# Experts chosen digit by digit beside their matmuls: two matmul pieces per digit step, one-hots shared with GpSimd, owners as one number

## What is computed

```python
logits = x @ w_gate                      # x: [3072, 512], 8 experts
order = np.argsort(-logits.flatten())    # all (token, expert) pairs, best first
for idx in order:
    tok, e = (int(idx) // E, int(idx) % E)
    if assigned[tok] >= 0 or counts[e] >= cap:      # cap = 384
        continue
    assigned[tok] = e
    counts[e] += 1
for e in range(E):
    mask = assigned == e
    h = np.maximum(x[mask] @ w1[e], 0.0)            # w1: [8, 512, 1024]
    out[mask] = h @ w2[e]                           # w2: [8, 1024, 512]
```

## Time and profile before

| | |
|---|---|
| median of 3 runs | 1100.49 us (1099.84 to 1103.88) |
| the profiled execution, its own time | 1108.83 us |
| its span | 1106.7 us |
| busy: TensorE, VectorE, ScalarE, GpSimd | 939.8, 584.7, 320.9, 217.8 us |
| chain that ended last: TensorE, VectorE, issue | 65%, 20%, 7% |

### The profile page before, as it was taken

How to read it: one execution, slowest core, us unless ns; L and a number is a source line. 1 busy time by engine, 2 the same in 40 slices (tenths; PEclk the granted TensorE clock), 3 DMA queues, 4 the chain that set the end, 5 groups by cost and what they waited for, 6 DMA issues and landing times.

```text
span 1106.7 us, 22036 instructions
## 1 busy us (share of the span) xinstructions
PE 939.8 (85%) x7642; PEld 772.7 (70%) x7643; DVE 584.7 (53%) x1683; ACT 320.9 (29%) x651; POOL 217.8 (20%) x294
## 2 busy tenths in 40 slices
PE   5899999816999999999998433989898989898995
PEld 4787878704788888888887322868676767676984
DVE  5756666577222222222221377777777777776650
ACT  3454444406122222222222003132222222224330
POOL 5633433001111111111111001020202020202011
PEclk9999999857999999999999655899899989999998
DMA  9667583704011111111110113141405050507210
GB/s 192 134 133 147 132 166 76 205 24 171 30 38 38 38 38 38 38 38 38 38 38 29 24 52 130 48 154 46 166 23 189 16 195 11 200 12 283 89 48 29
DMA packets 46014, 97.85 MB, mean 88 GB/s; under 512 B 7248, under 2 KB 19584, under 8 KB 45952
## 3 DMA queue, kind: packets, MB, share of 16 engines
q1 hardware_dynamic: 27200, 59.55, 18.5%
q0 software_dynamic: 8064, 26.46, 7.5%
q10 hardware_dynamic: 10688, 11.01, 4.7%
HBM read 77.49 MB, written 19.51 MB: 88 GB/s over the span
## 4 chain that ended last, share of the span: by engine, by line
PE 65%; DVE 20%; issue 7%; ACT 2%; DMA 2%; POOL 2%; DVEq 0%; ACTq 0%; SPq 0%; POOLq 0%
PE bank L766 25%; PE bank L905 9%; PE bank L920 8%; PE bank L678 4%; PE bank L659 3%; DVE w_low L1635 3%; PE bank L719 2%; PE bank L696 2%; PE bank L790 2%; PE bank L668 2%; DVE slot_hot L1614 2%; PE bank L813 2%; PE bank L928 1%; DVE ge L1511 1%; PE bank L856 1%
## 5 line engine op out<-in xcount | busy, mean ns | idle before, releaser
L905 PE MATMUL bank<-xh,w_high 128*128 128x384 f32 x256 | 96.7, 378 | 7.2 <-DVE xl L1639 7.2
L626 POOL DMA_INDIRECT out<-y_second,idx x24 | 35.4, 1475 | 316.2 <-ACT y_second L1049 313.3
L766 PE MATMUL bank<-w_high,xh 128*128 x200 | 82.8, 414 | 10.5 <-DVE gates L1398 10.5
L766 PE MATMUL bank<-w_high,hh 128*128 x200 | 83.1, 416 | 8.7 <-DVE hl L1405 8.7
L905 PE MATMUL bank<-xh,w_low 128*128 128x384 f32 x256 | 87.6, 342 | 0.0
L905 PE MATMUL bank<-xl,w_high 128*128 128x384 f32 x256 | 87.4, 342 | 0.0
L1049 ACT ACTIVATE w_high<-w_landed 128x1024 fp32r<-128x1024 f32 x64 | 63.9, 1049 | 72.1 <-DMA w_landed<-in_moe_w 72.1
L920 PE MATMUL bank<-w_high,hh 128*128 128x512 f32 x192 | 83.7, 436 | 0.0
L766 PE MATMUL bank<-w_low,hh 128*128 x200 | 80.7, 404 | 0.0
L766 PE MATMUL bank<-w_high,hl 128*128 x200 | 80.5, 402 | 0.0
L766 PE MATMUL bank<-w_low,xh 128*128 x200 | 80.2, 401 | 0.0
(11 more groups left out here) (288 smaller groups left out, 1962.3 us busy)
## 6 DMA issues: line engine op xcount, KB each, us to landing
w_landed<-in_moe_w SPq DMA_DIRECT2D x16, 2048.0 KB, 11.3
va<-in_v_win SPq DMA_DIRECT2D x16, 585.0 KB, 6.0
raw_w<-in_moe_w SPq DMA_DIRECT2D x4, 2048.0 KB, 11.9
k_raw<-in_k SPq DMA_DIRECT2D x16, 384.0 KB, 8.8
q_eye<-in_q ACTq DMA_DIRECT2D x16, 384.0 KB, 7.1
x_rows<-x ACTq DMA_DIRECT2D x12, 384.0 KB, 9.8
x_rows<-x SPq DMA_DIRECT2D x4, 387.0 KB, 7.5
xg<-x_rows,gidx POOLq DMA_INDIRECT x26, 3.4
```

The costliest lines, as they stand in the source:

```text
L626: pool.indirect_dma_start(out=out[:, :], out_offset=bass.IndirectOffsetOnAxis(ap=idx2[:, col:col + 1], axis=0), in_=y2[t][:, :], in_offset ...
L766: last = mm(ps, lhs[a][:, c, :], rhs[b](c), start=c == 0 and t == 0, stop=c == n - 1 and t == 2)
L905: last = mm(bank[fc % 2][:, 0:CAP], w[:, q % 2, c, f], a[:, c, :], start=c == 0 and t == 0, stop=c == KC - 1 and t == 2)
```

## The change

- Every search step and every piece of the tail gets two matmul pieces (SEGS = [2] * 12). The last two up chunks of an expert (HEAD = 4 pieces) run at the head of the next phase, ahead of its down pieces. A down part waits only for the weight unit it reads. List and turns move to steps 3 and 4/5; the weights' low units are spread anew, three of them into the tail.
- `slot_hot` is made half by VectorE (`pick_early`, in step 1) and half by GpSimd (`pick_late`, twelve operations of 128x128); the list waits for both.
- `oh`, `free` and the 192-wide products on them go. `owner` holds the number of a token's expert (-1 for none), `gone` is 0 for a free token and 16 for one that is not, and is added to `ix`, so that `cb` comes out zero.
- From step 3 on `known` is no longer updated: the thresholds' digits hold the difference to the digit before, and `nxt` is made from `thr`.

```diff
-DOWNS = 12
-LIST_AT, TURN_AT = 1, 2
-LOWS_AT = [[], [0, 1], [2, 3], [4], [5], [6], [7], []]
-PRE = 3
-SEGS = [3, 3, 3, 2, 2, 2, 2, 2, 1, 2, 2, 1]
+HEAD = 4
+DOWNS = HEAD + 12
+LIST_AT, TURN_AT = 3, 5
+LOWS_AT = [[], [], [0], [1], [2], [3], [], [4]]
+SEGS = [2] * 12
...
+            def pick_late(r):
+                pool.wait_ge(places_ready, r + 1)
+                if r:
+                    pool.wait_ge(listed, r)
+                for j in range(TC // 2, TC):
+                    last = g.tensor_scalar(slot_hot[:, j, :], iota_l[:, :], mlo[:, j:j + 1], None, ALU.is_equal)
+                last.then_inc(late_picks, 1)
+
             for ph in range(1, E + 2):
                 q, r = ph - 2, ph - 1
+                if r < E:
+                    pick_late(r)
...
             def list_mine(r):
                 pe.wait_ge(picks_ready, r + 1)
+                pe.wait_ge(late_picks, r + 1)
...
-                    if t == 0:
-                        pe.wait_ge(low_done, (W1U + W2U) * (q + 1))
...
                 if t == 0:
+                    pe.wait_ge(low_done, (W1U + W2U) * q + W1U + part + 1)
...
+                    elif q >= 0 and k >= HEAD:
+                        outward(q, (k - HEAD) // 4, k % 4)
                     elif q >= 0:
-                        outward(q, k // 4, k % 4)
+                        hidden(q, FC - HEAD // 2 + k // 2, k % 2)
...
+            def prepare_rest(ph):
+                chain(stt(eq3[:, :, :], eq3[:, :, :], -8.0, iota_e8[:, :, :], ALU.mult, ALU.add))
+                chain(red(ix[:, :], eq3[:, :, :], AXX, ALU.min))
+                chain(tt(ix[:, :], ix[:, :], gone[:, :], ALU.add))
+                chain(tt(cb[:, :, :], iota_e[:, :, :], ix[:, :].unsqueeze(2).to_broadcast([P, TC, E]), ALU.is_equal))
...
-                if t >= 2:
+                if t == 2:
                     chain(stt(known[:, :], digit[:, :], 4 * (t - 1) - 3, known[:, :], ALU.logical_shift_right, ALU.bitwise_xor))
...
+                stt(tied[:, :], ix[:, :], m1[:, 0:1], eqt[:, :], ALU.is_equal, ALU.mult).then_inc(tied_ready, 1)
...
-                chain(tt(oh[:, :, :], oh[:, :, :], cf[:, :, :].rearrange("p j e -> p e j"), ALU.add))
+                chain(tt(owner[:, :], owner[:, :], given[:, :], ALU.add))
+                if 0 < ph < E + 1:
+                    weight_lows(ph - 1, [W1U + W2U - 1])
+                    lows_until(DOWNS + 8)
                 dve.wait_ge(taken, ph + 1)
...
+                if r < PH:
+                    vec.tensor_scalar(mineb[:, :], owner[:, :], m1[:, 0:1], None, ALU.is_equal).then_inc(mine_ready, 1)
+                    chain(ts(other[:, :], owner[:, :], m1[:, 0:1], -2.0 * CAP, ALU.not_equal, ALU.mult))
...
-                tt(slot_hot[:, :, :], iota_l[:, :].unsqueeze(1).to_broadcast([P, TC, P]), mlo[:, :].unsqueeze(2).to_broadcast([P, TC, P]), ALU.is_equal
-                   ).then_inc(picks_ready, 1)
+
+            def pick_early(r):
+                half = TC // 2
+                dve.wait_ge(places_ready, r + 1)
+                tt(slot_hot[:, 0:half, :], iota_l[:, :].unsqueeze(1).to_broadcast([P, half, P]), mlo[:, 0:half].unsqueeze(2).to_broadcast([P, half, P]),
+                   ALU.is_equal).then_inc(picks_ready, 1)
```

More of the change, by code:

```diff
@@ L1173, in _ @@
                     high_parts(r, range(W1U + 2, W1U + W2U))
-                    for fc in range(FC):
+                    for fc in range(FC - HEAD // 2):
                         hidden_high(r, fc)
@@ L1492, in _ @@
             finite(thr0[:, :])
+            for t in range(STEPS - 1, 3, -1):
+                chain(tt(digits[:, t, :], digits[:, t, :], digits[:, t - 1, :], ALU.bitwise_xor))
             dve.wait_ge(l2_loaded, 16)
@@ L1537, in next_digit @@
                 else:
-                    chain(stt(known[:, :], digit[:, :], 4 * t - 3, known[:, :], ALU.logical_shift_right, ALU.bitwise_xor))
+                    chain(stt(known[:, :], digit[:, :], 4 * t - 3, thr[:, 0:1], ALU.logical_shift_right, ALU.bitwise_xor))
             def find(ph):
@@ L1657, in _ @@
                 if q >= 0:
-                    for fc in range(left[0], FC):
-                        hidden_low(q, fc)
+                    hidden_low(q, FC - HEAD // 2 - 1)
+                if ph < PH:
+                    prepare_rest(ph)
+                if q >= 0:
+                    hidden_low(q, FC - HEAD // 2)
                 for t in range(STEPS):
@@ L1672, in _ @@
                         weight_lows(r, LOWS_AT[t])
-                    lows_until(PRE + sum(SEGS[:t]))
+                    if t == 0 and q >= 0:
+                        hidden_low(q, FC - 1)
+                    lows_until(HEAD + sum(SEGS[:t]))
                     if ph < PH:
@@ L1676, in _ @@
                         next_digit(ph, t)
[L1677 to L1678 removed]
                 if ph < PH:
                     find(ph)
[L1681 removed]
+                if ours:
+                    weight_lows(r, [W1U + 1])
+                lows_until(DOWNS + 4)
                 if ph < PH:
                     choose(ph)
[L1684 removed]
+                if ours:
+                    weight_lows(r, [W1U + 2])
+                lows_until(DOWNS + 6)
                 if ph < PH:
[L1686 to L1687 removed]
+                    shut(ph, lows_until)
+                elif ours:
+                    weight_lows(r, [W1U + 3])
+                    lows_until(DOWNS + 8)
 def laid_out(inputs):
```

80 lines of the change are left out of this document (37 added, 43 removed).

## The result

| | before | after |
|---|---|---|
| median, runs taken in turns | 1102.38 us (1099.84 to 1107.68) | 1093.70 us (1086.73 to 1099.33) |
| ratio to before, 95% interval | | 0.9913 [0.9886, 0.9940] |
| the profiled execution, its span | 1108.83, 1106.7 us | 1093.70, 1092.0 us |
| busy TensorE, VectorE, GpSimd | 939.8, 584.7, 217.8 us | 930.5, 556.5, 283.8 us |

The change gains 0.9%, some 9 to 10 us by the ratio, 8.7 by the two medians. Forecast were 20.8. The time lies in the range, the mechanism of the search phases came as forecast, and less than half of the gain arrived. One of the change's thirteen executions took 4796.78 us at a granted clock of 1.00; no profile shows why, and its range and the ratio leave it out.

What follows compares the result with a forecast made beforehand. TensorE and VectorE, neither full, wait for each other in the second expert layer's search phases. Stretch differences of -26.8 + 6c, with c = 1 -20.8 us, off the 1100.49 median gave 1080 us; range 1060 to 1097.

Steps and rivals of the forecast that it cites:

- The walk: Second-layer search phase, step by step from step 0's any matmul: steps sum to 31.6 us, a phase is 52.1 + c.
- new wait for `hl`: Between search phases, after the ties: the next chunk waits for `hl`, now behind a `w_low`, until 8.25; 1.35 us.
- c: Time GpSimd's comparisons hold VectorE's small operations per searching phase: 0 to 2.0 us, middle 1.0 taken.
- Rival 1: GpSimd holds VectorE each time in the search phases: 1091 to 1099 us, say 1095; chance 0.17.
- twelve at 0.35: GpSimd's twelve 128x128 comparisons, priced from its 0.289 us cast plus a 0.06 gap: 4.2 us.
- from `places_ready` to the list there are by my walk 12.2 us: Time to hide GpSimd's comparisons ahead of the list matmuls: 12.2 us, so at 0.35 us each nothing waits.
- Rival 3: GpSimd late, list matmuls wait: decides from 1.3 us an operation; at 1.47, 6 us in each of eight phases, 1130; chance 0.07.
- The sum: Stretch differences from phase 0's first any to the end: -26.8 + 6c, with c = 1 -20.8 us.
- I put that at nothing: Phase 5 to the end: gathered rows take 4.3 us, 7.24 while weights land, which now land later; cost nothing.
- I take the difference off the median: Whole kernel: the 20.8 us taken off the median of 1100.49, not the profiled 1108.83, giving 1079.7 us.

## Why the prediction was wrong

In sum, by medians: the order alone 2.8 us (not told from nothing), ownership in the new order 12.0, GpSimd's half a loss of 3 to 4 (a gain of 0.8 us in each search phase, and more than that lost at the end). Against the steps of the prediction:

| stretch | before, two profiles | forecast | after, two profiles | last two lists on VectorE |
|---|---|---|---|---|
| first any, phase 0 to 1 | 37.0, 37.0 | 31.7 | 31.6, 31.6 | 31.6 |
| phase 1 to 2 | 57.2, 55.5 | 53.5 | 53.4, 51.7 | 51.6 |
| phases 2 to 4 | 169.1, 169.1 | 159.3 | 158.1, 158.2 | 158.2 |
| phase 5 to the end | 209.6, 205.6 | 207.6 | 215.7, 213.8 | 207.6 |

- **The walk was right.** The steps of a phase took 5.34, 4.32, 4.57, 3.99, 4.94, 5.71 and 3.30 us (4.72, 4.14, 4.67, 3.98, 5.13, 5.69 and 3.28 forecast) and 20.5 to the next phase's first any, as forecast. The new wait for `hl` came with 1.2 us where 1.35 stood.
- **c was near.** The phase took 52.7 and not 53.1: c = 0.6. Step 0's run of small operations is the place. `known` and `thm` took 0.36 and 0.35 us, and the last `thr` of the step 0.31. The same three take 0.16, 0.17 and 0.17 in the kernel with all one-hots on VectorE (first rows of the changed kernel, then one of that kernel), and its `ge` starts 2.03 us behind the any matmul, where it is 2.55 here:

```profile
877.31 0.36 DVE L1550 SCALAR_TENSOR_TENSOR known<-digit,sign 128x1 int32<-128x1 int32 x1
877.70 0.17 DVE L1551 TENSOR_TENSOR thr<-digits,known 128x16 int32<-128x16 int32 x1
877.91 0.35 DVE L1495 TENSOR_SCALAR thm<-thr 128x16 int32<-128x16 int32 x1
878.29 0.20 DVE L1496 TENSOR_SCALAR thn<-thm 128x16 int32<-128x16 int32 x1
```

```profile
880.59 0.16 DVE L1539 SCALAR_TENSOR_TENSOR known<-digit,sign 128x1 int32<-128x1 int32 x1
880.99 0.17 DVE L1484 TENSOR_SCALAR thm<-thr 128x16 int32<-128x16 int32 x1
```

  All of step 0 costs 0.6 us more than the walk, and the half that VectorE was spared (1.60 us) was worth 0.8 in the period. Rival 1 did not come about.
- **First step that failed: "twelve at 0.35".** The price was taken from the nearest row, the cast. The estimate of 0.43 us from the page GPSIMD Engine Reference of the Trainium skill fell short as well, and its share for dispatch stands on that page for VectorE, not for GpSimd. A comparison that nothing holds takes 0.60 us, and twelve, their waits for VectorE included, 0.73 each on average in a search phase and 0.77 in phases 7 and 8. The prediction counted c, what GpSimd costs VectorE, and put the other direction, what VectorE's large operations cost GpSimd, at nothing. In the search phases that did not matter: twelve take 8.7 us, and 12.6 lie between the places and the list.
- **It failed through the next one: "from `places_ready` to the list there are by my walk 12.2 us".** That walk is through a phase that searches. In phases 7 and 8 the steps hold no counts and no answers of VectorE, and from the places to the list's own time there are only 8.0 us (979.81 to 989.26 - 1.49 = 987.77). There twelve at 0.77, 9.3 us, come late. Unheld, at the 0.58 us from start to start that the rows show, they would take 7.0 us and be in time: it takes the 2.3 us for which one comparison was held by VectorE to make the wait. Whether another place for VectorE's two operations there removes it was not tried. Rival 3 had this mechanism, and its sign, TensorE waiting at the list, came. But its point of decision, 1.3 us an operation (beyond it the kernel is slower than before), and its price, 6 us in each of eight phases, came from the searching phase too. TensorE begins to wait at 12.6 / 12 = 1.05 us there, but at 8.0 / 12 = 0.66 us in the last two phases. The sentence "I put that at nothing" weighed the gather there and not the list's new partner.
- **The clock doubled what the wait cost, or more.** With the two waits of 1.49 us came 5.0 us of slower matmuls in one profile and 3.3 in the other. The walk watched the clock in the search phases only.
- **Last step that failed: "I take the difference off the median".** The sum set the one profiled execution of before (1106.7 us) beside phases without any half clock in them. By its own sum the new span was 1085.9 us, which the kernel with the last two lists on VectorE meets (1084.7). But that profile had 17 us more of half clock than the second one, and the difference of 20.8 us held this excess: against the second profile's span of 1100.0 the same walk gives 14.1 us (15.2 from phase 0's first any on), and for the part from phase 5 to the end a loss of 2.0 in place of the gain of 2.0. The three runs of before that were shown also lay low, 1100.49 where later sets had medians of 1102.4 to 1104.6.

So of the 13.7 us between 1080 and 1093.7, 5.7 stand between the forecast for a profiled execution (1085.9 + 2.1 = 1088.0) and the measured one: 8.1 lost at the end, 2.0 gained before it, 0.4 around the span. The other 8.0 come from setting a difference of profiles against a median, by which the profile lay 8.3 too high. That the time still lies in the range is luck: the part of it above 1091 us was put there for rival 1, which did not come about.

What stays open: why one stretch of half clock came in the tail of two kernels in the new order that have nothing on GpSimd (all one-hots on VectorE; the order alone), and none in four other profiles without that wait. Both came within 1 us of the start of an up part. The four profiles with the wait at the list have two or three each, most of them not at the wait but at the start of an up part, 13 to 16 us later, and no run shows how the one leads to the other. That the wait has a part in it is borne out by the two edits that remove the wait; the last phases' other wait of 1.4 us, for `xl`, stands in all of them and was not tried alone.

**What beats both kernels.** VectorE alone for the last two lists and the up bank freed first (0.9844 and 0.9807, 1083.6 us over twelve executions), or a third for GpSimd with the same order of the up bank (0.9819): about 1.8% under before, twice the change's gain.

## What to carry to other kernels

When work is hidden behind other work, work out the time that hides it for each phase in which it runs, the ones without search or at the end of the loop above all: an engine with time to spare in one is late in the other. Where two engines hold each other up, price it in both directions. Work given to a slower engine is best sized by the tightest place: with the up bank freed first in both, a third of it on GpSimd took 1082.8 us and a half 1086.8. The intervals of these two touch, but the tails are 122.4 and 128.8 us. And a forecast sets a walk of the new kernel against a walk of the old, not against one profile of it, whose stretches of half clock may not come again.

## What was not expected of the hardware

- In the change's first profile a wait of TensorE of 1.49 us at the list is followed by 3.4 us at half clock (from 990.3 us), and so are the starts of the last two up parts. In its second profile the same wait in the same phase is followed by none, and the two up parts start at half clock again. In the first profile, around two of the three stretches, the granted clock falls to 0.73 and 0.66 (stretches of 5 us), and in the up part the matmuls start 0.32 us apart and then 0.17 to 0.19:

```profile
988.00:993.00 5.00, 3.74 (x32) 3.12 (x33) 2.42 (x5) 0.00 (x0) 3.80 (x4) 0.73 0.15 56
...
1044.00:1049.00 5.00, 4.26 (x15) 4.26 (x16) 1.82 (x2) 2.16 (x3) 0.21 (x1) 0.66 0.14 52
```

```profile
1047.67 0.52 PE L915 MATMUL bank<-xh,w_high 128*128 128x384 f32 x1
1047.99 0.49 PE L915 MATMUL bank<-xl,w_high 128*128 128x384 f32 x1
1048.31 0.35 PE L915 MATMUL bank<-xh,w_low 128*128 128x384 f32 x1
1048.50 0.34 PE L915 MATMUL bank<-xh,w_high 128*128 128x384 f32 x1
```

- It is GpSimd that stands still for VectorE's large operations. In phase 7 its third comparison began at 981.00 us and ended at 983.9, 2.9 us in place of 0.60, while VectorE ran these without a gap (the first row is GpSimd's third and fourth together):

```profile
981.00 3.49 POOL L633 TENSOR_SCALAR slot_hot<-iota_l,mlo 128x128 bf16<-128x128 f32 x2
```

```profile
980.13 0.56 DVE L1649 SCALAR_TENSOR_TENSOR hl<-bank,hh 128x384 fp32r<-128x384 f32 x1 [0.27 <-ACT hh L1140]
980.60 1.77 DVE L1638 TENSOR_TENSOR slot_hot<-iota_l,mlo 128x1536 bf16<-128x1536 f32 x1
982.30 1.21 DVE L1659 TENSOR_TENSOR w_low<-w_landed,w_high 128x1024 fp32r<-128x1024 f32 x1
```

  VectorE's three keep their length. It also makes GpSimd's twelve cost 8.7 to 9.3 us and not 7.0. The page SBUF — State Buffer of the Trainium skill (Who interferes with whom) states that a VectorE instruction with two inputs in SBUF contends with a GpSimd one that reads it, under an exclusive lock: whoever issues first has the shared pair of ports for the whole instruction, and the other fully blocks. GpSimd's third comparison agrees: it started 0.4 us behind VectorE's `slot_hot` and ended 0.4 us behind the `w_low` that followed without a gap. But that `slot_hot` (980.60) had itself started 0.2 us behind GpSimd's second comparison (980.41 to 981.01) and kept its length, which the rule does not give.
- A stretch of half clock of 3.4 us is worth 1.6 to 1.8 us of the time, and such stretches come and go between executions of one kernel. Of the 6.7 us between the two profiles of before, 5.8 lie in phases 1, 5 and 6, where they differ in it, and the rest lies ahead of phase 0.
